# A fused attention, expert and gated-FFN kernel: operand sets of six up blocks made during the expert steps and kept in DRAM, a new order of units, and out weights split piece by piece

## The chip, the cores and the metric

The kernel runs on one core of a Trainium2 chip. A core has a matmul engine (TensorE, PE in the profile), VectorE (DVE), ScalarE (ACT), GpSimd (POOL) and SyncE (SP), which here only issues DMAs. The time is that of one launch in device microseconds; the runs shown give 937.08 us as the median of three (935.49 to 937.7).

## The reference

```
attn: phi(x) = [exp(p), exp(-p)], p = x @ w_phi - max|x @ w_phi|;  out = phi(q) (phi(k)^T v) / (phi(q) sum phi(k))
x     = attention's rows, 2304 x 512
moe:  e = argmax(x @ w_gate);  x = gate_w * sigmoid(x @ w_output_gate)[e] * (relu(x @ w1[e]) @ w2[e])
ffn:  xn = x / rms(x) * rms_g;  out = (silu(xn @ w_gate) * (xn @ w_val)) @ w_out       (512 -> 1536 -> 512)
```

Everything is float32. TensorE takes an operand as a rounded high part and a low part (`fp32r`), and each product of matrices is three matmuls: high by high, high by low and low by high.

## The kernel before, in words

Attention is first, the experts second. With these inputs the expert phase has eight steps of 288 rows on three experts. A step has eight chunks m of hidden rows: `hidden(m)` on TensorE, `relu` on ScalarE (the high part), `relu_low` on VectorE, and `outputs(m - 2)`. At the chunk m = 7 the rows of the next step are turned (`next_transpose`, four pieces) and split (`take_rows` on ScalarE and VectorE). `copy_out`, `add_squares`, `mean`, `root`, `inverse` and `normal` normalise a step's rows during the next step, and SP stores them into `xn_dram`. The first steps of an expert also split the next expert's weights.

The FFN's up part makes 12 blocks of 128 hidden columns for three groups of 768 rows, in 36 units (one block, one group). A unit is one two-by-two product made with seven products instead of eight; each product has six matmuls of 384 columns, so a unit has 42. For this the block's weights need four given parts and three sums, and a group's rows too. GpSimd makes the sums (`up_sums`, `up_last_sum`, `row_sums`), ScalarE rounds the high parts (`up_high`, `row_high`), VectorE subtracts for the low parts (`up_low`, `row_low`). TensorE does `product(u, 0)`, `(u, 1)`, `(u, 2)`, then the last product of unit u - 1, then `(u, 3)` to `(u, 5)`. ScalarE copies three sums per unit from PSUM (`first_copy`, L1418, before product 3 may start; `second_copy`, L1424, before product 5; `third_copy`, L1430, when product 5 is done) and computes two sigmoids (`first_sigmoid`, L1408; `second_sigmoid`, L1412). VectorE adds the gates and values and multiplies; SP stores the result (`hidden_out`, 384 KB).

A block's weights are loaded raw (512 KB, `up_in`, L568) into one of three staging buffers and split again each time the block comes up: 14 loads, in two operand buffers (`tH_up`, `tL_up`). Units go: blocks 0 and 1 with group 0, 0 and 1 with group 1, blocks 2 to 9 with all three groups each, blocks 10 and 11 by group, and blocks 0 and 1 again with group 2. Each engine's queue is an order written out by hand; an engine runs its queue in order, so whoever waits holds up all that stands behind it. SP's queue is one queue for loads and stores.

At the end the FFN's out weights (`out_high`, L1436; `out_low`, L1960) are split in two lumps of six, and 18 tiles of 128 rows are loaded, split and multiplied (L1188 to L1190).

Of the kernel before, what the change touches and what calls it, by code (L numbers as in the profile page):

```python
# [51 lines left out]
NQ = NF + 2  # L52
NT = NTOK // P
UNITS = ([(q, sg) for sg in range(2) for q in range(2)] + [(q, sg) for q in range(2, NF - 2) for sg in range(NSG)]
         + [(q, sg) for sg in range(NSG) for q in (NF - 2, NF - 1)] + [(NF, NSG - 1), (NF + 1, NSG - 1)])
NU = len(UNITS)


def unit_block(u):
    return UNITS[u][0] % NF  # L60


def first_of_pair(q):
    return min(u for u in range(NU) if UNITS[u][0] == q)


def last_of_pair(q):
    return max(u for u in range(NU) if UNITS[u][0] == q)
# [6 lines left out]
def last_of_group(sg):  # L75
    return max(u for u in range(NU) if UNITS[u][1] == sg)

# [5 lines left out]
def build_program(nc, q, k, v, w_phi, wg, wog, w1, w2, ffn_up, ffn_out, rms_g, out):  # L83
# [4 lines left out]
    xn_dram = nc.dram_tensor("xn_dram", [P, KC, NTOK + G], F32).ap()  # L88
    h_dram = nc.dram_tensor("h_dram", [P, NT, NF, P], F32).ap()
    ids_dram = nc.dram_tensor("ids_dram", [NTOK + G, 1], F32).ap()  # L90
    ctx = ExitStack()
    with ctx:
# [68 lines left out]
        put = placer(at_raw, RAW)  # L161
        tH_up, tL_up = [None, None], [None, None]
        tH_up[1] = put("upH1", [P, 7, 2, P], F32R)
        tL_up[1] = put("upL1", [P, 7, 2, P], F32R)
        xst = [put("xst0", [P, KC, 2 * GN]), None, None]
        xst[2] = xst[0]
        w_st = [put("w_st0", [P, 6, 2, P]), None, None]
        put = placer(at_work + 30368, WORK - 30368)
        tH_up[0] = put("upH0", [P, 7, 2, P], F32R)
        tL_up[0] = put("upL0", [P, 7, 2, P], F32R)  # L170
# [5 lines left out]
        w_st[1] = placer(at_work + 20032, 6144)("w_st1", [P, 6, 2, P])  # L176
        ysb = placer(at_work + 20032, 6144)("ysb", [P, 3, DM])

        PIECE = 2 * GN * 4

        def piece(n, count=1):
            return placer(at_set0 + n * PIECE, count * PIECE)

        own = ([*range(0, 10), *range(22, 26)], [*range(10, 22), 26, 27], [*range(28, 42)])
        sH = [[piece(own[sg][2 * o])(f"sH{sg}_{o}", [P, 2, GN], F32R) for o in range(7)] for sg in range(NSG)]
# [246 lines left out]
        def staging_of(q):  # L432
            return (0, 2)[q] if q < 2 else 1 - q % 2

        def loads_of(q):

            return 16 * len([n for n in range(q + 1) if staging_of(n) == staging_of(q)])
# [1642 lines left out]
```

## Time and profile before

| | us |
|---|---|
| median of 3 runs | 937.08 |
| the profiled execution, its own time | 927.2 |
| its span, first to last instruction | 925.6 |
| PE busy | 851.8 (92%) |
| DVE / ACT / POOL busy | 530.2 / 359.0 / 197.6 |
| DMA moved | 95.41 MB, mean 103 GB/s |

"Busy" is an average over stages. The digits of the page's second part show where TensorE isn't busy: slices of 23 us each, digits in tenths.

### The profile page before, as it was taken

The page shows a single profiled execution, that of the slowest core. Times are in us where ns is not written, and L with a number is a line of the kernel's source. Part 1 is how long each engine was busy: PE and PEld are TensorE (multiplying, and loading weights), DVE is VectorE, ACT ScalarE, POOL GpSimd, SP SyncE. Part 2 cuts the span into 40 slices and gives each one's busy share as a digit, 9 for nine tenths or more (in the row PEclk, how much of TensorE's full clock was granted, in tenths as well). Part 3 has the DMA queues.
Part 4 walks back from the last instruction along what each step waited for, and adds up shares of the span by engine and source line. Part 5 has one row for each costly group of instructions (what it writes and reads, how often), then busy time and mean ns, then how long its engine had stood idle before and what let it go on. Part 6 is the DMA issues. An engine that isn't in the chain of part 4 may idle for free.

```text
span 925.6 us, 16649 instructions
## 1 busy us (share of the span) xinstructions
PE 851.8 (92%) x6216; PEld 769.6 (83%) x6217; DVE 530.2 (57%) x931; ACT 359.0 (39%) x607; POOL 197.6 (21%) x211
## 2 busy tenths in 40 slices
PE   8999999999999999998672899999999678999997
PEld 6776868589999999998562799999999677888886
DVE  5688888998576333226664766666675484221220
ACT  4545555651454222224521543443443343222221
POOL 1011202034432122234604211111120120111011
PEclk9999999999999999999885999999999879999999
DMA  8615523023573212253007122222231623433430
GB/s 282 185 53 209 180 95 109 1 79 91 196 231 56 34 43 30 47 142 112 21 8 158 43 74 75 75 84 81 75 97 52 248 70 115 136 132 130 137 103 34
DMA packets 59755, 95.41 MB, mean 103 GB/s; under 512 B 8848, under 2 KB 42768, under 8 KB 57648
## 3 DMA queue, kind: packets, MB, share of 16 engines
q1 hardware_dynamic: 55392, 75.99, 28.5%
q0 software_dynamic: 3488, 17.85, 5.2%
q8 instruction: 37, 0.61, 0.3%
q10 hardware_dynamic: 816, 0.79, 0.3%
q14 instruction: 22, 0.18, 0.1%
HBM read 61.55 MB, written 33.08 MB: 102 GB/s over the span
## 4 chain that ended last, share of the span: by engine, by line
PE 76%; DVE 11%; issue 5%; DMA 3%; ACT 3%; POOL 1%; SPq 0%; POOLq 0%; ACTq 0%; DVEq 0%
PE ps L1138 8%; PE ps L1140 7%; PE ps L1139 7%; PE ps L1188 5%; PE ps L1190 5%; PE ps L1189 5%; PE ps L1049 4%; PE ps L1050 4%; PE ps L1051 4%; PE ps L1062 4%; PE ps L1064 4%; PE ps L1063 4%; PE ps L890 3%; PE ps L945 2%; PE ps L850 2%
## 5 line engine op out<-in xcount | busy, mean ns | idle before, releaser
L1138 PE MATMUL ps<-sH,upH 128*128 128x384 f32 x504 | 178.5, 354 | 53.9 <-ACT part L1424 28.7
L1139 PE MATMUL ps<-sL,upH 128*128 128x384 f32 x504 | 175.7, 349 | 0.0
L1140 PE MATMUL ps<-sH,upL 128*128 128x384 f32 x504 | 175.5, 348 | 0.0
L1138 PEld LDWEIGHTS ps<-sH,upH 128*128 128x128 f32 x504 | 99.7, 198 | 59.6 <-ACT part L1424 30.8
L1139 PEld LDWEIGHTS ps<-sL,upH 128*128 128x128 f32 x504 | 99.7, 198 | 0.1
L1140 PEld LDWEIGHTS ps<-sH,upL 128*128 128x128 f32 x504 | 99.4, 197 | 0.0
L1966 DVE TENSOR_TENSOR hTL<-h_st,hTH 128x768 fp32r<-128x768 f32 x36 | 32.9, 954 | 97.7 <-ACT hTH L1446 97.7
L1188 PE MATMUL ps<-woH,hTH 128*128 128x512 f32 x216 | 84.1, 389 | 2.4 <-DVE hTL L1966 2.4
L1742 DVE SCALAR_TENSOR_TENSOR hmL<-ps,hmH 128x288 fp32r<-128x288 f32 x64 | 29.2, 456 | 96.4 <-ACT hmH L1293 91.7
L1189 PE MATMUL ps<-woL,hTH 128*128 128x512 f32 x216 | 84.0, 389 | 0.0
L1190 PE MATMUL ps<-woH,hTL 128*128 128x512 f32 x216 | 84.0, 389 | 0.0
L1049 PE MATMUL ps<-xmH,w1H 128*128 128x288 f32 x256 | 76.0, 297 | 3.9 <-issue 2.0
L1062 PE MATMUL ps<-hmH,w2H 128*128 128x288 f32 x256 | 78.6, 307 | 0.0
L1050 PE MATMUL ps<-xmL,w1H 128*128 128x288 f32 x256 | 76.1, 297 | 0.0
L1051 PE MATMUL ps<-xmH,w1L 128*128 128x288 f32 x256 | 76.0, 297 | 0.0
L1064 PE MATMUL ps<-hmH,w2L 128*128 128x288 f32 x256 | 75.7, 296 | 0.0
L1063 PE MATMUL ps<-hmL,w2H 128*128 128x288 f32 x256 | 75.6, 296 | 0.0
L1293 ACT ACTIVATE hmH<-ps 128x288 fp32r<-128x288 f32 x64 | 26.3, 411 | 114.6 <-PE ps L1064 93.9
L1540 DVE TENSOR_REDUCE mx<-ps 128x4 f32<-128x512 f32 x72 | 49.2, 684 | 17.9 <-PE ps L852 17.7
L1547 DVE TENSOR_TENSOR pm<-ps,mx 128x512 f32<-128x512 f32 x72 | 49.8, 691 | 5.4
L1049 PEld LDWEIGHTS ps<-xmH,w1H 128*128 128x128 f32 x256 | 48.2, 188 | 4.7 <-issue 4.7
L1452 ACT ACTIVATE ysb<-ps 128x512 f32<-128x512 f32 x18 | 10.8, 598 | 105.8 <-PE ps L1190 105.8
(238 smaller groups left out, 1782.5 us busy)
## 6 DMA issues: line engine op xcount, KB each, us to landing
h_dram<-hid SPq DMA_DIRECT2D x36, 384.0 KB, 2.7
h_st<-h_dram SPq DMA_DIRECT2D x18, 768.0 KB, 4.2
w_st<-in_ffn_up SPq DMA_DIRECT2D x14, 512.0 KB, 4.5
xin<-xs_dram SPq DMA_DIRECT2D x9, 578.2 KB, 8.2
xs_dram<-zrow SPq DMA_DIRECT2D x8, 578.2 KB, 7.6
qT<-in_q SPq DMA_DIRECT2D x4, 1152.0 KB, 6.1
xn_dram<-x2g SPq DMA_DIRECT2D x8, 576.0 KB, 5.5
xst<-xn_dram SPq DMA_DIRECT2D x3, 1536.0 KB, 8.6
```

What stands on the lines that cost most here:

```text
L1049: e.matmul(o, w1H[par][:, c, cols], xmH[:, c, :], start=(c == 0), stop=False)
L1050: e.matmul(o, w1H[par][:, c, cols], xmL[:, c, :], start=False, stop=False)
L1051: last = e.matmul(o, w1L[par][:, c, cols], xmH[:, c, :], start=False, stop=(c == KC - 1))
L1062: e.matmul(o, w2H[par][:, m, cols], hmH[:, m % 2, :], start=(m == 0), stop=False)
L1063: e.matmul(o, w2H[par][:, m, cols], hmL[:, m % 2, :], start=False, stop=False)
L1064: last = e.matmul(o, w2L[par][:, m, cols], hmH[:, m % 2, :], start=False, stop=(m == FC - 1))
L1138: e.matmul(to, wh, xh, start=(fresh and c == 0), stop=False, skip_group_check=True)
L1139: e.matmul(to, wh, xl, start=False, stop=False, skip_group_check=True)
L1140: done = e.matmul(to, wl, xh, start=False, stop=(c == 1), skip_group_check=True)
L1188: e.matmul(to, hi, woH[:, i, :], start=(i == 0), stop=False, skip_group_check=True)
L1189: e.matmul(to, hi, woL[:, i, :], start=False, stop=False, skip_group_check=True)
L1190: done = e.matmul(to, lo, woH[:, i, :], start=False, stop=(i == NF - 1), skip_group_check=True)
```

## The change

An up block's operands, 1.75 MB with high and low parts, become a "set" in one of three buffers `tb[v % 3]`. A list `VISITS` names the block of each of 16 visits.

- Expert steps: each step after the first loads a block's raw weights (512 KB), makes three sums on GpSimd, one high part of 1792 elements on ScalarE (behind relu 5) and one low part on VectorE (behind relu_low 6), and SP stores the set (1.75 MB) to `t_dram`. With eight steps, steps 1 to 6 are stored: blocks 0 to 5. The last step makes a set that isn't stored.
- Up part: visits of blocks 0 to 5 load their set in two DMAs (1 MB, 0.75 MB). Six visits (6, 7, 8, 10, 11, 12) still load raw weights, into one staging buffer `w_st`, and make the set at units 11, 14, 17, 19, 22, 25 (`MADE_AT`).
- Order: units 0 to 3 are blocks 0 to 3 with group 0, units 4 to 6 blocks 1 to 3 with group 1, then blocks 4 to 8 with all groups, block 0 with groups 1 and 2, blocks 9 to 11 by group, and blocks 1 to 3 with group 2. Row operands are placed between copies by a table (`ROWS_AT`).
- Out weights are split one piece at a time from unit 30 on, and tile 0's rows in unit 34; their loads are issued at units 26 and 29.
- After the experts the sum of squares stands before product 2 of unit 1, and the root's function table is loaded once before all sigmoids.

```diff
+VISITS = (0, 1, 2, 3, 4, 5, 6, 7, 8, 0, 9, 10, 11, 1, 2, 3)
+MADE = (6, 7, 8, 10, 11, 12)
+MADE_AT = {6: 11, 7: 14, 8: 17, 10: 19, 11: 22, 12: 25}
+OUT_AT = {(30 + (n + 1) // 3, "ABC"[(n + 1) % 3]): n for n in range(NF)}
...
 (SP, in the loop over expert steps)
+                step_weights_in(n + 1)
                 rows_out(n)
+                weights_out(n + 1)
...
+            def step_weights_in(n):
+                e.wait_ge(s["e_st"], n * 16 + 16)
+                e.dma_start(t_raw[:, 0:4, :, :].rearrange("p o c n -> p (o c n)"), ffn_up[nth]...).then_inc(s["e_in"], 16)
+            def weights_out(n):
+                e.wait_ge(s["e_lo"], n + 1)
+                e.dma_start(t_dram[nth]..., tb[1][:, :, :, :, :]...).then_inc(s["e_st"], 16)
+            def weights_in(v):
+                if nth_made(v) > 0:
+                    e.wait_ge(s["t_lo"], 2 * nth_made(v))
+                else:
+                    e.wait_ge(s["s_lo"], 7 * NSG)
+                e.dma_start(w_st[:, 0:4, :, :]..., ffn_up[VISITS[v] + 1]).then_inc(s["w_in"], 16)
...
             for u in range(2, NU):
                 hidden_out(u)
+                for vis in range(4, len(VISITS)):
+                    if vis not in MADE and last_of_visit(vis - 3) == u + 1:
+                        operands_in(vis)
+                    if vis == MADE[0] and u == 8 or vis in MADE[1:] and u == MADE_AT[MADE[nth_made(vis) - 1]]:
+                        weights_in(vis)
...
 (ScalarE)
+            def weights_high(g):
+                e.wait_ge(s["e_add"], g * 3 + 3)
+                e.activation(tb[1][:, 0, :, :, :], t_raw[:, :, :, :], ACT.Copy).then_inc(s["e_hi"], 1)
+            def made_high(v, half):
+                slots, free = (slice(0, 4), slice(4, 7))[half], ("pe_U", "pe_D")[half]
+                e.wait_ge(s["t_add"], 3 * nth_made(v) + 3)
+                e.wait_ge(s[free], last_of_visit(v - 3) + 1)
+                e.activation(tb[v % 3][:, 0, slots, :, :], w_st[:, slots, :, :], ACT.Copy).then_inc(s["t_hi"], 1)
+            for u in range(2, NU):
                 first_copy(u)
                 first_sigmoid(u)
+                beside(u, "A")
                 second_sigmoid(u - 1)
                 second_copy(u)
+                beside(u, "B")
                 third_copy(u)
+                beside(u, "C")
```

Three places of ScalarE's queue follow. First, the second half of an expert step, before; `hmH` is a relu, `xmH` the next step's rows:

```order
L1293 ACTIVATE hmH<-ps 128x288
L1291 REGISTER_ALU
L1293 ACTIVATE hmH<-ps 128x288
L1286 ISA
L1287 ACTIVATE xmH<-ps 128x288
```

and in the changed kernel:

```order
L1380 ACTIVATE hmH<-ps 128x288
L1401 ISA
L1403 ACTIVATE tb_94<-t_raw 128x1792
L1378 REGISTER_ALU
L1380 ACTIVATE hmH<-ps 128x288
L1373 ISA
L1374 ACTIVATE xmH<-ps 128x288
```

The set's high part stands between relu 5 and relu 6, behind a wait for GpSimd. Second, the start of the up part, before (`upH` are weights, `sH` rows, `part` the copies, `hid` the sigmoids):

```order
L1310 ACTIVATE mx<-ones 128x1
L1384 ACTIVATE upH_97<-w_st_96 128x768
L1456 REGISTER_ALU
L1402 ACTIVATE sH_0_109<-xst_95 128x768
L1402 ACTIVATE sH_1_110<-xst_95 128x768
L1402 ACTIVATE sH_2_111<-s_sum_2_151 128x768
L1384 ACTIVATE upH_97<-w_st_96 128x768
L1418 ACTIVATE part_104<-ps 128x384
```

and in the changed kernel:

```order
L1486 ACT_TABLE_LOAD
L1486 ACTIVATE sH_0_109<-xst_97 128x768
L1486 ACTIVATE sH_1_110<-xst_97 128x768
L1486 ACTIVATE sH_2_111<-s_sum_2_151 128x768
L1486 ACTIVATE sH_3_112<-s_sum_3_152 128x768
L1384 ISA
L1386 ISA
L1388 ACTIVATE x2g<-ps 128x1152
L1502 ACTIVATE part_106<-ps 128x384
```

The weight operands are gone from the front; a table load is still there. Third, units 17 to 19 of the changed kernel, with the made sets of visit 8 (`tb_95`) and visit 10 (`tb_94`):

```order
L1473 ACTIVATE tb_95<-w_st 128x768
L1514 ACTIVATE part_108<-ps 128x384
L1502 ACTIVATE part_106<-ps 128x384
L1492 ACTIVATE hid_103<-gate_0_101 128x384
L1496 ACTIVATE hid_104<-gate_1_102 128x384
L1508 ACTIVATE part_107<-ps 128x384
L1514 ACTIVATE part_108<-ps 128x384
L1502 ACTIVATE part_106<-ps 128x384
L1492 ACTIVATE hid_104<-gate_1_102 128x384
L1473 ACTIVATE tb_94<-w_st 128x1024
L1496 ACTIVATE hid_103<-gate_0_101 128x384
L1508 ACTIVATE part_107<-ps 128x384
```

Only one unit, 18, lies between the two made sets; between the others lie two.

## Rows read from the trace of the kernel before

**Rows 1.** The page's slices of the span, TensorE's busy tenths.
```profile
PE   8999999999999999998672899999999678999997
```
**Rows 2.** Timeline of PE: start, us, line, what, idle time before it and its releaser.
```profile
435.03 0.44 PE L1138 MATMUL ps<-sH,upH 128*128 128x384 f32 x1 [3.51 <-DVE sL L1928]
...
448.25 0.69 PE L1138 MATMUL ps<-sH,upH 128*128 128x384 f32 x1 [2.58 <-DVE upL L1916]
...
453.60 0.34 PE L1140 MATMUL ps<-sH,upL 128*128 128x384 f32 x1
...
771.71 0.50 PE L1188 MATMUL ps<-woH,hTH 128*128 128x512 f32 x1 [2.44 <-DVE hTL L1966]
```
**Rows 3.** Timeline of ACT: third copies of units 6, 7, 31 and 35.
```profile
534.68 0.49 ACT L1430 ACTIVATE part<-ps 128x384 f32<-128x384 f32 x1 [1.32 <-PE ps L1140]
...
541.99 0.49 ACT L1430 ACTIVATE part<-ps 128x384 f32<-128x384 f32 x1 [1.59 <-PE ps L1140]
...
719.32 0.49 ACT L1430 ACTIVATE part<-ps 128x384 f32<-128x384 f32 x1 [1.59 <-PE ps L1140]
...
769.31 0.49 ACT L1430 ACTIVATE part<-ps 128x384 f32<-128x384 f32 x1
```
**Rows 4.** Timeline of SP's queue: stores of two steps' rows, a raw block's load.
```profile
396.56 0.62 SPq L547 DMA_DIRECT2D xn_dram<-x2g  x1
...
423.80 0.62 SPq L547 DMA_DIRECT2D xn_dram<-x2g  x1
...
487.86 0.35 SPq L568 DMA_DIRECT2D w_st<-in_ffn_up  x1
```
**Rows 5.** Timeline of ACT: the two waits for a load.
```profile
497.70 0.84 ACT L1384 ACTIVATE upH<-w_st 128x768 fp32r<-128x768 f32 x1 [18.43 <-DMA w_st<-in_ffn_up]
...
733.48 2.19 ACT L1436 ACTIVATE woH<-wo_st 128x512 fp32r<-128x512 f32 x4 [8.38 <-DMA wo_st<-in_ffn_out]
```
**Rows 6.** Timeline of SP's queue: a raw block is asked for after unit 31.
```profile
719.73 0.54 SPq L568 DMA_DIRECT2D w_st<-in_ffn_up  x1
```
**Rows 7.** Timeline of POOL: sums of 256 and 768 elements.
```profile
414.26 0.73 POOL L777 TENSOR_TENSOR w_st<-w_st 128x256 f32<-128x256 f32 x1
...
425.85 1.84 POOL L793 TENSOR_TENSOR s_sum<-xst 128x768 f32<-128x768 f32 x1 [9.36 <-PE ps L1051]
...
724.05 0.74 POOL L777 TENSOR_TENSOR w_st<-w_st 128x256 f32<-128x256 f32 x1 [28.96 <-DMA w_st<-in_ffn_up]
...
726.33 1.33 POOL L780 TENSOR_TENSOR w_st<-w_st 128x256 f32<-128x256 f32 x1
```
**Rows 8.** Timeline of ACT: the last expert step, the junction, unit 32's first sigmoid.
```profile
424.16 0.41 ACT L1293 ACTIVATE hmH<-ps 128x288 fp32r<-128x288 f32 x1 [2.81 <-PE ps L1064]
...
430.05 1.28 ACT L1310 ACT_TABLE_LOAD   x1 [1.15 <-issue]
...
431.46 0.83 ACT L1384 ACTIVATE upH<-w_st 128x768 fp32r<-128x768 f32 x1
...
442.11 0.41 ACT L1384 ACTIVATE upH<-w_st 128x256 fp32r<-128x256 f32 x1
...
722.38 0.52 ACT L1408 ACTIVATE hid<-gate 128x384 f32<-128x384 f32 x1 [1.51 <-DMA h_dram<-hid]
```
**Rows 9.** Timeline of DVE: the last expert step, and row operands beside GpSimd and alone.
```profile
426.40 0.82 DVE L1736 TENSOR_TENSOR xmL<-ps,xmH 128x288 fp32r<-128x288 f32 x2 [1.34 <-ACT xmH L1287]
...
441.87 2.40 DVE L1928 TENSOR_TENSOR sL<-s_sum,sH 128x768 fp32r<-128x768 f32 x1 [0.38 <-ACT sH L1402]
...
479.13 0.95 DVE L1928 TENSOR_TENSOR sL<-xst,sH 128x768 fp32r<-128x768 f32 x1
```
**Rows 10.** DMA issues of the window 395 to 545 us: count, size each, median us to landing.
```profile
xst<-xn_dram SPq DMA_DIRECT2D x3, 1536.0 KB, 8.6
...
xin<-xs_dram SPq DMA_DIRECT2D x1, 578.2 KB, 8.3
```
**Rows 11.** The stores into `xn_dram` (576 KB each), by that name: all eight.
```profile
DMA to landing us min/median/max: 3.4/5.6/13.6
```

More of the change, by code:

```diff
@@ L284, in build_program @@
             "normalised, stored; token numbers stored, read": "dve_xn xst idst id_in id_c",
+            "FFN up weights of a step: loaded, sums, operands split, stored": "e_in e_add e_hi e_lo e_st",
             "FFN rows loaded (one per group), their sums, operands split": "x_in0 x_in1 x_in2 s_add s_hi s_lo",
-            "FFN up weights loaded (one per staging buffer), their sums, operands split":
-                "w_in0 w_in1 w_in2 t_add t_hi t_lo",
+            "FFN up operands loaded (two parts per buffer)": "t_a0 t_a1 t_a2 t_b0 t_b1 t_b2",
+            "FFN up weights loaded, their sums, operands split (two parts each)": "w_in t_add t_hi t_lo",
             "a unit's products: the first, the second, sixth added, fifth added, fourth added": "pe_F pe_A pe_U pe_V pe_D",
@@ L431, in build_program, with step_number, nth_load, nth_made @@
         BANKS = ((2, 7, 0, 1), (3, 4, 5, 6))
[L432 to L437, printed above, removed]
-        def before_in_staging(q):
-            return max([n for n in range(q) if staging_of(n) == staging_of(q)], default=None)
+        SLOT = (0, 3, 2, 1, 5, 4, 6)
+        def step_number(g):
+            return nc.s_assert_within(g, 0, NSTEP - 1, skip_runtime_bounds_check_because="there are at most NSTEP steps")
+        def nth_load(v):
+            return len([n for n in range(v + 1) if n % 3 == v % 3 and n not in MADE])
+        def nth_made(v):
+            return MADE.index(v)
         def stores_of(u):
@@ L1777, in _ @@
                 take_rows(0, XT_FIRST)
-                for name in ("dve_ms", "dve_R", "dve_xn"):
+                for name in ("dve_ms", "dve_R", "dve_xn", "e_lo"):
                     e.sem_inc(s[name], 1)
@@ new lines, in beside @@
+            def beside(u, pos):
+                before = slot_before(u, pos)
+                if before in ROWS_AT:
+                    row_low(*ROWS_AT[before])
+                for vis in MADE:
+                    if before[0] == MADE_AT[vis] and before[1] != "C":
+                        made_low(vis, "AB".index(before[1]))
+                if before in OUT_AT:
+                    out_low(OUT_AT[before])
+                if before in TILE0_AT:
+                    tile_rows_low(0, TILE0_AT[before])
@@ new lines, in _ @@
+            for o in range(4):
+                row_low(0, o)
+            first_gate(0)
+            for o in range(4, 7):
+                row_low(0, o)
+            values(0)
+            first_gate(1)
+            mean(total - 1, BANKS[1][3])
+            second_gate(0)
+            inverse(total - 1)
+            hidden_rows(0)
+            values(1)
+            normal(total - 1)
+            for u in range(2, NU):
+                first_gate(u)
+                beside(u, "A")
+                second_gate(u - 1)
+                beside(u, "B")
@@ L2008, in _ @@
                 hidden_rows(u - 1)
                 values(u)
[L2010 to L2022 removed]
+                beside(u, "C")
@@ L2034, in _ @@
-                if u == NU - 1:
-                    for half in range(2):
-                        tile_rows_low(0, half)
             second_gate(NU - 1)
```

430 lines of the change are left out of this document (193 added, 237 removed).

## Prediction

> **What bounds the kernel now.** I read the slices first [rows 1]: TensorE is at 8 or 9 tenths everywhere but in two dents, slices 19 to 23 (the junction from the experts to the up part) and 32 to 34 (where the out weights come in). So the end is set by TensorE's work plus what it loses in the two dents, and what a change is worth there is read from the waits there.
>
> How much is lost: the third copies, one per unit right behind the unit's last sum, are a ruler [rows 3]. Units 6 and 7 lie 541.99 - 534.68 = 7.31 us apart, the length of an undisturbed unit (42 matmuls of 0.174). The experts' matmuls end at 435.03 - 3.51 = 431.5 [rows 2]. Unit 7's third copy could come eight units later, less the one product that is made in the next unit (1.04) and plus 0.1: 489.1. It comes at 541.99: 52.9 us are lost at the junction. From unit 7 to 31 it takes 177.3 for 24 x 7.31 = 175.4: 1.9 lost. From 31 to 35, 50.0 for 29.2: 20.8 lost. The first tile then waits 2.4 [rows 2]. In all 78.0 us.
>
> What the waits are: at the front TensorE waits 3.5 for VectorE's first low parts of rows. Its restart at 448.25 after 2.58 idle runs on the low level of the clock, 1.2 GHz: the 16 matmuls from there to 453.60 take 5.35 us, where 0.174 each and 0.25 for a restart make 3.0: 2.3 us lost [rows 2]. I use 2.3 for each wait of over 2.5 us. The largest is 18.4 us of ScalarE for block 2's raw weights [rows 5]: their load is issued only at 487.86 [rows 4], since in SP's queue it stands behind the store of the last normalised rows, with nothing for TensorE to do. In the second dent ScalarE waits 8.4 us for the out weights [rows 5] with copies queued behind it.
>
> **The change, part by part.**
>
> *Junction.* Four units on group 0 (29 us of work) now stand before group 1, and nine units (66 us) before group 2; blocks 0 to 3 come ready from DRAM. The 18.4 us wait and those for later groups have no cause left, if the loads come. Chain at the front: the table load at 430.05 stays, so the first high part of rows starts where `upH` starts now, 431.46, takes 0.83, and VectorE's low part 0.95 alone [rows 8, 9]: TensorE starts at about 433.35, 1.85 late instead of 3.5. Product 4 of unit 0 waits for its low part beside `add_squares` on GpSimd, where such a subtraction takes up to 2.40 instead of 0.95 [rows 9]: 0.7, and product 5 again 0.6. In unit 1 the matmuls of the squares take 0.3, and ScalarE has a root with its table, another table (1.28 each [rows 8]) and two sigmoids before the second copy: 1.0. In unit 2 VectorE is behind by `inverse` and `normal`: 0.6. One more for units 3 to 8, where row operands are slotted in. Sum 6.05, all short waits, so I put no clock on them: 6.0 instead of 52.9.
>
> The loads behind this: a set of 1.75 MB is 1.17 times a group of rows, 1536 KB in 8.6 us [rows 10], so about 10 us alone. Sets 1 and 2 are asked for at about 427.5 and 428.5, group 1 at 431.5, set 3 at 436 and 442. Even one after the other at 8 to 10 us each they are there at 437, 446, 455 and 463, where unit 1 starts at 441, unit 2 at 449, unit 3 at 457 and group 1 (unit 4) at 464. Set 3 is behind group 1 and would be late by up to 6 us on this count; but landing times include a fixed part that overlapped DMAs don't pay again, so I take 0 and keep 6 + 2.3 for a rival.
>
> *Expert steps.* Per step GpSimd gets sums of 512, 256 and 256 elements: 1.28 (between 0.73 for 256 and 1.84 for 768 [rows 7]) + 0.73 + 0.73 = 2.8. ScalarE gets 1792 elements: 0.41 for 256 and 0.83 for 768 [rows 8] give 1.67, in the 2.8 us that it waits between two relus [rows 8]: covered. VectorE gets 1792 x 0.95 / 768 = 2.2 at most, from 425.1 on, half a us behind ScalarE's relu 6 [rows 8]: it runs to 427.2, over the place of the next rows' low parts at 426.40 [rows 9], which then end 0.7 later, and TensorE's third and fourth transposes need those. I find 0.2 of stall per step, seven steps, 1.4; in the two steps that also split the next expert's weights there is less room, 0.8 each: 3.0. Bounds: 0 (the relus have several us of slack), and 2.2 x 7 = 15.4 if each subtraction passes whole.
>
> The ring `t_raw`, sums, high, low, store, next load must fit a step of 27.2 (the stores of two steps' rows, 396.56 and 423.80 [rows 4]). Store 1.75 MB: from 9 us (group load, scaled) to 17 (the 576 KB store of 5.6 [rows 11] times 3.1); load 4.3 [rows 6, 7]; 2.8; 1.7; 2.2: 20 to 28. I take 20, since the stored rows are long pieces as in the group's load, and the 576 KB store has short ones. The rows' load of 8.3 us [rows 10] stands behind the store, and is still there before GpSimd gates it.
>
> By the Trainium skill (DMA: Bandwidth & Descriptors, Anatomy of one DMA) a DMA's semaphore waits for the receipt of the last byte from the target memory, which takes longest for HBM; this speaks for the long end of the ring. The store of 576 KB at 5.6 us [rows 11] agrees with a slow store; by that rule alone the expert term would be larger by the rival B below.
>
> *Middle.* A set made in the up part needs: load issued at the end of unit E, sums, then the high part in slot A of a later unit. Now: issue 719.73, about 0.5 behind unit 31's end (719.2); sums from 724.05 to 727.66 [rows 6, 7]. So 8.5 behind the end; with 512 elements in the first sum 9.0. Slot A of the next unit is right behind the first sigmoid, 722.90 [rows 8], 3.7 behind the end; of the one after, 11.0. All sets but one are asked for two units ahead: 2.0 to spare. Visit 10 is asked for behind unit 18 and made in unit 19, with slot A at 3.7: ScalarE waits 5.3, then the high part of 1024 elements (1.0), the second sigmoid and the second copy (0.45 each): the copy is ready 11.0 behind the end of unit 18, where product 5 of unit 19 wants it at 6.3 (six products of 1.05). TensorE loses 4.7 and 2.3 for the clock, 7.0. Bounds 0 and 9.3. The 1.9 of small things stays.
>
> On the clock the Trainium skill (TensorE: Matmul & The Clock Gate, Part 1) says that the number of cold matmuls varies between runs of one kernel. The rows above show 16; by the rule the 7.0 would be anything from 4.7 up to 7.0.
>
> *Second dent.* Out weights are asked for at unit 26 (3 MB) and split one by one from unit 30, 0.55 and 0.62 us each, in gaps: ScalarE's and VectorE's work per unit grows to 4.2 and 5.9 of 7.31. Tile 0 is split in unit 34. What is left: the stores of hidden rows queue behind the 3 MB, and a first sigmoid waits for such a store already (1.51 [rows 8]): 1.5. Instead of 20.8 + 2.4. Bounds 0 and 8.
>
> *Sum.* Lost after: 6.0 + 1.9 + 7.0 + 1.5 + 3.0 = 19.4; before 78.0. Gain 58.6. The profiled execution 927.2 - 58.6 = 868.6. The median shown is 9.9 us or 1.07% above that execution; in proportion this gives 878.
>
> **The rivals.**
>
> A. As summed: 878 us.
>
> B. The ring or VectorE's subtraction reaches into each step. For it: VectorE is at the transposes' limit; for seven steps nothing catches up. Against: the slack of the relus. 2 to 3 us more per step, or a set that is late at the junction (8.3): 878 + 17 = 895.
>
> C. Visit 10 is in time, or the wait is swallowed: for it, sums alone take 2.8 instead of 3.6. Against: even that gives the copy at 0.5 + 4.3 + 2.8 + 1.0 + 0.9 = 9.5, where 6.3 is due; it needs more. 878 - 7 = 871, with no cost in the steps 868.
>
> D. Slower: the ring decides the step. From 27.2 us on each us goes into six steps; the gain is eaten when the ring takes 37 us, that is when store and load together land 30 us after issue. If the store scales like the slowest of its kind (13.6 us for 576 KB [rows 11] would be 42), the ring is 53 and the time 878 + 6 x 26 = 1034. Against: the store's long rows.
>
> E. It doesn't do what it says: the waits only move from the weights to the rows, since sums, splits and stores of the last step stay as they are. If half of what I take off the junction stays (23.5), 902; if all stays, no change, 937.
>
> **How the numbers follow.** A 0.52, B 0.22, C 0.15, D 0.03, E 0.08 (of which 0.01 no change). The time is A's, 878. The range takes B and C in and stops before E: 863 to 898. A measurement of this kernel can tell about 0.2% from no change. Faster 0.95, same 0.01, slower 0.04.
>
> **What would show it.** In the changed profile: a slice row without the first dent; the third copies 7.3 apart from unit 2 on but for one gap of 14 at unit 19, with ScalarE's longest wait "DMA w_st" or "POOL w_st" there; relus in the expert steps still 3.2 apart and steps of 27.2; the first matmul of the up part 1.9 behind the last of the experts; the first tile's matmul right behind unit 35. Steps of over 28 us would show B; matmuls waiting for `tb` loads, a late queue; a junction with waits for `sL`, E.

## The result, and the profile after

The changed kernel takes 901.87 us (median of 4 runs, 901.04 to 903.25) where the kernel before takes 936.29 (932.16 to 937.7): ratio 0.9641, 95% interval 0.9607 to 0.9674. It is faster, by 34.4 us and not by the 59 forecast, and 901.9 lies outside the range of 863 to 898. Its profiled execution took 903.25 us, with a span of 901.5.

The page's slices of the changed kernel (TensorE, then its granted clock) answer to [rows 1]:

```profile
PE   8999999999998899999898899998999999999997
PEclk9999999999999999999989999998999999999999
```

The two dents are gone as deep ones; what is left are single tenths at many places: slices 13, 14 and 17 in the expert steps, 20, 22 and 23 around the junction, 28 at units 19 and 20. Who is waited for, in PE's waits (us in all, times, longest):

```profile
PE ps L1225 <- ACT part L1508: 14.5, 8, 3.8
PE ps L1225 <- DVE sL L1991: 7.0, 4, 3.4
PE ps L1098 <- DVE xmL L1792: 3.7, 2, 2.4
```

The largest is the second copy of a unit, eight times, none longer than 3.8. Such a list names only the last link, so I go by the ruler of [rows 3] again. ScalarE's timeline has the first table load, with which the expert steps begin, and the third copies of units 7, 31 and 35; PE's has the first matmul of the up part:

```profile
245.64 1.28 ACT L1397 ACT_TABLE_LOAD   x1 [2.77 <-issue]
526.35 0.49 ACT L1514 ACTIVATE part<-ps 128x384 f32<-128x384 f32 x1 [0.68 <-PE ps L1227]
712.96 0.49 ACT L1514 ACTIVATE part<-ps 128x384 f32<-128x384 f32 x1 [1.06 <-PE ps L1227]
747.84 0.49 ACT L1514 ACTIVATE part<-ps 128x384 f32<-128x384 f32 x1 [1.59 <-PE ps L1227]
```

```profile
448.98 0.45 PE L1225 MATMUL ps<-sH,tb 128*128 128x384 f32 x1 [1.88 <-DVE sL L1991]
```

The experts end at 448.98 - 1.88 = 447.10. Unit 7 could come 57.5 us later (the count of the prediction), at 504.6, and comes at 526.35: 21.7 lost. From 7 to 31 it takes 186.6 for 175.4, from 31 to 35 34.9 for 29.2. From the table load to the experts' end it takes 201.5 us; before it was 431.5 - 238.4 = 193.1. Term by term:

| us lost | predicted | profile after |
|---|---|---|
| junction, to unit 7 | 6.0 | 21.7 |
| small things, units 8 to 31 | 1.9 | 2.8 |
| visit 10 at units 19 and 20 | 7.0 | 6.5 |
| second dent (unit 29: 1.9, units 32 and 33: 5.7) | 1.5 | 7.6 |
| expert steps | 3.0 | 8.4 |
| sum | 19.4 | 47.0 |

Before's second profile (b0_again below) has 194.5 us of expert steps instead of 193.1, and five profiles of after have 199.4 to 202.5, so the 8.4 is 5 to 9.

What each of them is, in the timelines. The rows of the expert steps come first: VectorE's low part of the six blocks, then its low part of the next step's rows, for which TensorE's last transposes wait.

```profile
301.01 2.01 DVE L1931 TENSOR_TENSOR tb<-t_raw,tb 128x1792 fp32r<-128x1792 f32 x1
302.94 0.81 DVE L1792 TENSOR_TENSOR xmL<-ps,xmH 128x288 fp32r<-128x288 f32 x2
303.53 0.96 PE L1098 MATMUL ps<-ident,xin 96*128 96x96 f32 x6 [2.37 <-DVE xmL L1792]
```

Unit 0, at the junction, loses 7.0 us: its third copy comes 13.3 us behind the experts' end instead of 6.4. TensorE waits 1.88, 1.17 and 0.52 us for low parts of rows, while VectorE works beside GpSimd's last sum of group 0 (1.82 us alone, 2.59 here). And it runs on the low level of its clock: 18 matmuls start 0.32 us apart, where 0.174 is usual. The last line is the stretch of 447 to 461 us (busy times, then granted clock 0.76, DMA share, GB/s):

```profile
448.04 2.59 POOL L886 TENSOR_TENSOR s_sum<-xst 128x768 f32<-128x768 f32 x1
447.97 3.47 DVE L1991 TENSOR_TENSOR sL<-xst,sH 128x768 fp32r<-128x768 f32 x2 [2.88 <-issue]
451.50 0.69 PE L1225 MATMUL ps<-sH,tb 128*128 128x384 f32 x1 [1.17 <-DVE sL L1991]
447.00:461.00 14.00, 10.43 (x42) 9.13 (x42) 11.71 (x9) 7.70 (x12) 8.93 (x5) 0.76 0.85 295
```

Over the whole junction (447.10 to 526.35) TensorE stands idle for 13.0 us, and 49 matmuls are 0.32 us apart instead of 0.174. That is about 7 us (estimate: 49 x 0.146), so a third of the 21.7 is the clock.

Unit 2 loses 5.1: GpSimd's sums of group 1 stand beside VectorE's hidden rows and normalisation, and ScalarE waits for a gate behind them. VectorE's multiplication of hidden rows, 0.96 us alone, takes 2.48, and the normalisation's four instructions take 3.90.

```profile
467.40 2.67 POOL L882 TENSOR_TENSOR s_sum<-s_sum,xst 128x768 f32<-128x768 f32 x1
468.40 2.48 DVE L2019 TENSOR_TENSOR hid<-hid,val 128x768 f32<-128x768 f32 x1
471.86 3.90 DVE L1819 SCALAR_TENSOR_TENSOR x2g<-x2g,gcol,rinv 128x288 f32<-128x288 f32 x4
476.26 0.52 ACT L1492 ACTIVATE hid<-gate 128x384 f32<-128x384 f32 x1 [6.41 <-DVE gate L1997]
478.36 0.69 PE L1225 MATMUL ps<-sH,tb 128*128 128x384 f32 x1 [2.96 <-ACT part L1508]
```

Unit 4: SyncE asks for row group 2 (1536 KB) at 481.00, and the 384 KB store of unit 2's hidden rows follows at 488.62. ScalarE's first sigmoid of unit 4 may only overwrite that buffer once the store has landed, 7.1 us later; such a store takes 2.9 us in the median. The last line is the busy share, in tenths, of the DMA engines from 486 to 497 us, in slices of 0.275:

```profile
481.00 0.58 SPq L628 DMA_DIRECT2D xst<-xn_dram  x1
488.62 11.64 SPq L633 DMA_DIRECT2D h_dram<-hid  x2
495.76 0.52 ACT L1492 ACTIVATE hid<-gate 128x384 f32<-128x384 f32 x1 [5.72 <-DMA h_dram<-hid]
498.15 0.41 PE L1225 MATMUL ps<-sH,tb 128*128 128x384 f32 x1 [3.41 <-DVE sL L1991]
DMA  9999996310000999990000000000000000000000
```

The load isn't what the store waits for: the load lands 7.7 us after its issue, at 488.7, as the store is issued. The store's packets move from 489.6 to 491.2, then the engines are all but idle until it counts as landed at 495.76. Between load and store stands one more DMA, in every kernel here: the store of the last step's token numbers (`ids_dram`, 1.1 KB in pieces of 4 B, issued at 481.93), which itself lands late (10.7 us in a0_again). In before the hidden store issued right behind it (485.22 and 485.88) took 11.0 us, the longest of all there. Whether it delays the hidden stores was not tested.

Unit 6 isn't such a case either. ScalarE waits 4.83 us there, but the store is issued only at 511.53, 3.2 us behind unit 5's third copy (508.36), since VectorE is late beside GpSimd's sums of group 2, and it lands in 3.1 us like any other.

```profile
511.53 0.37 SPq L633 DMA_DIRECT2D h_dram<-hid  x1
514.72 0.52 ACT L1492 ACTIVATE hid<-gate 128x384 f32<-128x384 f32 x1 [4.83 <-DMA h_dram<-hid]
```

Unit 32 is a store behind loads: a set (`tb`) and two tiles' hidden rows (`h_st`) stand before it, the DMA engines are busy all the time, and it lands after 8.0 us. Unit 29, behind the 3 MB of out weights, is the smaller case (6.5 us).

```profile
705.99 4.39 SPq L614 DMA_DIRECT2D tb<-t_dram  x2
710.51 0.99 SPq L643 DMA_DIRECT2D h_st<-h_dram  x2
712.97 0.37 SPq L633 DMA_DIRECT2D h_dram<-hid  x1
721.07 0.52 ACT L1492 ACTIVATE hid<-gate 128x384 f32<-128x384 f32 x1 [6.58 <-DMA h_dram<-hid]
722.95 0.44 PE L1225 MATMUL ps<-sH,tb 128*128 128x384 f32 x1 [3.78 <-ACT part L1508]
```

Unit 19 is the wait that was predicted: the raw weights of visit 10 are asked for at the end of unit 18, and ScalarE waits 4.38 for their sums.

```profile
609.57 0.54 SPq L624 DMA_DIRECT2D w_st<-in_ffn_up  x1
617.12 1.06 ACT L1473 ACTIVATE tb<-w_st 128x1024 fp32r<-128x1024 f32 x1 [4.38 <-POOL w_st L873]
619.02 0.69 PE L1225 MATMUL ps<-sH,tb 128*128 128x384 f32 x1 [3.56 <-ACT part L1508]
```

### The profile page after: what moved, and what is told of

Same layout as the page of the kernel before. It is cut to its first block, busy times and chain, and to the rows that moved or that the text cites. A ratio compares the mean times of both kernels' runs of the same rounds, so it can differ in the third digit from the quotient of the medians.

```text
span 901.5 us, 16661 instructions
## 1 busy us (share of the span) xinstructions
PE 851.4 (94%) x6216; PEld 767.9 (85%) x6217; DVE 527.1 (58%) x908; ACT 354.3 (39%) x583; POOL 186.0 (21%) x194
## 4 chain that ended last, share of the span: by engine, by line
PE 76%; DVE 10%; issue 6%; DMA 4%; ACT 2%; POOL 0%; DVEq 0%; POOLq 0%; SPq 0%; ACTq 0%
PE ps L1225 8%; PE ps L1227 7%; PE ps L1226 7%; PE ps L1277 5%; PE ps L1276 5%; PE ps L1275 5%; PE ps L1133 4%; DMA h_dram<-hid 4%; PE ps L1134 3%; PE ps L1135 3%; PE ps L1146 3%; PE ps L1148 3%; PE ps L1147 3%; PE ps L974 3%; PE ps L1029 3%
## 5 line engine op out<-in xcount | busy, mean ns | idle before, releaser
L1225 PE MATMUL ps<-sH,tb 128*128 128x384 f32 x504 | 175.6, 348 | 23.2 <-ACT part L1508 14.5
L1227 PE MATMUL ps<-sH,tb 128*128 128x384 f32 x504 | 173.4, 344 | 0.0
L1226 PE MATMUL ps<-sL,tb 128*128 128x384 f32 x504 | 173.2, 344 | 0.0
L1225 PEld LDWEIGHTS ps<-sH,tb 128*128 128x128 f32 x504 | 97.9, 194 | 28.8 <-ACT part L1508 21.1
L1226 PEld LDWEIGHTS ps<-sL,tb 128*128 128x128 f32 x504 | 97.8, 194 | 0.1
L1227 PEld LDWEIGHTS ps<-sH,tb 128*128 128x128 f32 x504 | 97.5, 193 | 0.0
L1380 ACT ACTIVATE hmH<-ps 128x288 fp32r<-128x288 f32 x64 | 26.3, 411 | 105.0 <-PE ps L1148 84.2
L904 POOL DMA_INDIRECT out_dram<-ysb,idI x18 | 17.4, 967 | 219.1 <-ACT ysb L1536 219.1
## 6 DMA issues: line engine op xcount, KB each, us to landing
t_dram<-tb SPq DMA_DIRECT2D x6, 1792.0 KB, 11.1
xin<-xs_dram SPq DMA_DIRECT2D x9, 578.2 KB, 11.4
```

The source lines that it names most:

```text
L1225: e.matmul(to, wh, xh, start=(fresh and c == 0), stop=False, skip_group_check=True)
L1226: e.matmul(to, wh, xl, start=False, stop=False, skip_group_check=True)
L1227: done = e.matmul(to, wl, xh, start=False, stop=(c == 1), skip_group_check=True)
```

## The experiments

All times are in this table: medians with the lowest and highest run, the ratio to the kernel before with its 95% interval, and from each profile the ruler's losses (junction, units 8 to 31, second dent from unit 31 on) and the length of the expert steps. Kernels of one set ran on one chip; the difference to "after" counts within a set.

| set, kernel | us | ratio to before | steps | junction | 8 to 31 | from 31 |
|---|---|---|---|---|---|---|
| 0 after | 901.9 (901.0 to 903.3) | 0.964 (.961 to .967) | 201.5 | 21.7 | 11.2 | 5.6 |
| 1 after (a0) | 892.5 (890.9 to 893.2) | 0.956 (.953 to .959) | 200.0 | 15.8 | 9.0 | 5.7 |
| 1 stores on ScalarE's queue (e1) | 916.2 (913.5 to 920.6) | 0.983 (.979 to .987) | 199.3 | 26.3 | 14.0 | 12.7 |
| 1 visits 6, 7, 8 sooner (e4) | 896.8 (894.5 to 897.7) | 0.961 (.958 to .964) | 200.7 | 18.2 | 8.1 | 6.4 |
| 2 after (a1) | 899.1 (896.2 to 903.0) | 0.964 (.959 to .968) | 199.4 | 20.8 | 12.0 | 6.1 |
| 2 visit 8 sooner (e4b) | 898.9 (896.3 to 902.8) | 0.962 (.959 to .965) | 202.2 | 21.0 | 12.8 | 5.7 |
| 2 no row sums (e5) | 895.1 (892.9 to 896.3) | 0.958 (.955 to .961) | 201.0 | 14.9 | 10.7 | 6.7 |
| 2 loads in pieces (e6) | 890.8 (887.7 to 891.4) | 0.953 (.950 to .957) | 201.6 | 17.8 | 8.8 | 0.9 |
| 3 after (a2) | 898.5 (893.6 to 900.3) | 0.961 (.958 to .964) | 202.5 | 16.6 | 11.9 | 6.0 |
| 3 low parts behind rows (e2) | 893.4 (888.3 to 895.0) | 0.956 (.952 to .959) | 195.6 | 18.3 | 9.3 | 5.5 |
| 3 raw loads one unit sooner (e9) | 889.5 (887.6 to 890.6) | 0.952 (.950 to .955) | 200.4 | 16.8 | 3.2 | 5.4 |
| 3 four edits (e12) | 875.0 (874.5 to 879.8) | 0.939 (.937 to .942) | 195.6 | 16.0 | 1.4 | 0.2 |
| 4 after (a3) | 894.4 (893.9 to 897.7) | 0.956 (.954 to .959) | 199.8 | 17.4 | 9.3 | 7.6 |
| 4 3 KB stores (e13) | 895.7 (891.8 to 896.6) | 0.957 (.953 to .961) | 200.4 | 15.9 | 6.4 | 6.6 |
| 4 four edits (e12b) | 878.9 (875.5 to 881.4) | 0.941 (.937 to .944) | 195.6 | 16.3 | 1.3 | 0.3 |
| 4 four edits, 3 KB stores (e14) | 876.2 (872.4 to 878.2) | 0.936 (.932 to .939) | 195.7 | 14.8 | 0.9 | 0.7 |
| 5 e1 with 3 KB stores (e15) | 892.5 (889.9 to 896.2) | 0.957 (.954 to .960) | 199.9 | 21.8 | 7.0 | 4.8 |
| 5 e12 with these (e17) | 883.7 (881.5 to 887.1) | 0.948 (.944 to .952) | 195.7 | 18.7 | 6.0 | 2.8 |

**The same kernels again.** The attention stage, whose code is unchanged, was 7.3 us longer in the profile after.

> The kernel before, unchanged, profiled a second time. In the two profiles the expert steps begin at 238.4 us (before) and 245.6 us (after), though the attention stage is the same code. Theory 'chance': the attention stage differs from one execution to the next, so the expert steps begin here anywhere from 238 to 246 us, and the profiled execution takes 927 to 937 us. Rival 'the change costs 7 us in the attention stage' (another layout of the program): they begin at 238 to 239 us again and the profiled execution takes about 927 us.

> The kernel after, unchanged, profiled and timed a second time. Theory 'chance': the expert steps begin somewhere from 238 to 246 us, the rest of the profile (expert steps 200 us, junction 21.5 us lost, second dent 7.5 us lost) repeats within 1 us each; time 902. Rival 'the change costs 7 us in the attention stage': they begin at 245 to 246 us again.

The kernel before, profiled again, took 934.87 us, and its expert steps begin at 244.66:

```profile
244.66 1.28 ACT L1310 ACT_TABLE_LOAD   x1 [2.76 <-issue]
```

In the profiles of the kernel after they begin at 245.6, 243.4, 243.4, 245.5 and 245.9, in all other kernels below between 243.3 and 248.4. So the 7 us aren't the change, and the profile of before that the prediction rests on was a short one. The kernel after itself is less steady than I expected: medians of 892.5 to 901.9 us in five sets of runs, each spread over 2 to 7 us, where before has medians of 932.4 to 936.3 in six.

> The kernel after once more, on the same chip as the three kernels sent with it. It took 901.9 us in one set of runs and 892.5 us in another. Theory 'sets of runs differ': anywhere from 890 to 903 us, and the gaps between third copies at units 4, 6, 19, 29 and 32 repeat within 2 us each. Rival 'one of the two sets was an exception': 892 us again.

> The kernel after once more, for the comparison with the three kernels sent with it. It has taken 892.5, 899.1 and 901.9 us in three sets of runs, while the kernel before took 933.6, 934.0 and 936.3. All theories: 890 to 903 us.

> The kernel after, for the comparison with the three kernels sent with it: 890 to 903 us by all theories.

The part that differs most is the junction (15.8 to 21.7), and next the second expert step (28.5 to 31.4 us; before has 27.2 and 28.6). In the junction 2.5 us are unit 0: its third copy comes 13.3 us behind the experts' end in after and a1_again, and 10.8 in the other three. There GpSimd's last sum of group 0 is over as VectorE begins, TensorE's two further waits of 1.17 and 0.52 are one of 0.51 to 0.55, and 14 to 16 matmuls run on the low level of the clock instead of 18. So one profile of each kernel can't tell a difference of 2 or 3 us at the junction.

**Hidden stores on another queue (e1).** The store and its wait move from SyncE's queue to ScalarE's:

```
 second_sigmoid(u - 1) ... third_copy(u); beside(u, "C")
+hidden_out(u - 1)          # was SyncE's
```

> After, with the stores of the hidden rows issued on ScalarE's queue, behind the third copy, instead of on SyncE's, where they stand behind loads of 0.8 to 1.8 MB. Theory 'one queue': ScalarE's waits for a hidden store at units 4, 6, 29 and 32 (5.7, 4.8, 5.0, 6.6 us) shrink to the 3 us that a store takes alone, and with them PE's losses there (4.3, 2.5, 1.9 and 5.7 us): 888 to 892 us. Rival 'the DMA engines themselves are full': the stores land as late from another queue, since the same 16 engines carry the loads: 899 to 903 us. Second rival 'the loads are only the last of several lateness': the store lands early, but VectorE is late there (it runs beside GpSimd), and PE waits as long for another engine: 895 to 902 us.

All three accounts missed: 916.2 us, 23.7 slower than after in its set. The load of group 2 in SyncE's queue, the store, and what waits for it:

```profile
473.36 0.57 SPq L628 DMA_DIRECT2D xst<-xn_dram  x1
474.23 0.38 ACTq L1489 DMA_DIRECT2D h_dram<-hid  x1
486.79 0.52 ACT L1484 ACTIVATE hid<-gate 128x384 f32<-128x384 f32 x1 [10.26 <-DMA h_dram<-hid]
488.89 0.69 PE L1217 MATMUL ps<-sH,tb 128*128 128x384 f32 x1 [7.59 <-ACT part L1506]
```

Issued 0.9 us behind one load, the store lands 12.5 us later, worse than any in SyncE's queue (at most 8.8 in five profiles of after). "One queue" falls: another queue is no way past a load. The Trainium skill says as much (DMA: Bandwidth & Descriptors, Issuing engines are not separate DMA queues): DMAs run on the same 16 DMA engines and interleave, whoever starts them. The trace agrees. But e1 changes an order too. This is unit 1's store, which SyncE's queue issues 0.6 us ahead of the load in after (480.40 and 481.00), where it lands in 3.3 us; with the store on ScalarE's queue nothing holds the load back for it. The 23.7 us are the price of the other queue and of the order that came with it, and no run separates the two.

**Loads in pieces (e6).** If the bytes under way count, fewer at a time help:

```
-group_in(2)
+group_in(2, rows 0:2) ... hidden_out(2); group_in(2, rows 2:4)
-unit 26: wo_st thirds 0, 1, 2      unit 29: hidden_in(0), hidden_in(1)
+units 26, 27, 28: one third each   units 32, 33: one tile each
```

> After, with SyncE's large loads spread among the hidden stores: row group 2 in two halves (before and behind the store of unit 2), the out weights in thirds at units 26, 27 and 28 instead of all at 26, the first two tiles' hidden rows at units 32 and 33 instead of both at 29. Theory (formed after the store from ScalarE's queue had landed 12.5 us late beside one load): a 0.4 MB store takes as long as the bytes that are under way with it, so only fewer bytes at a time help; losses at units 4, 29, 32 and 33 fall from about 10 us to 3 us: 6 to 7 us below the kernel after of this call. Rival 'the bytes are the same and the queue is full anyway': within 1.5 us of the kernel after.

890.8 us, 8.3 less than after in its set, and no run of the one overlaps one of the other. Unit 32's third copy follows 7.6 us after unit 31's instead of 12.6, unit 29's 7.3 instead of 9.3; unit 4 gains only 0.9 (12.2 to 11.3). The first sigmoid of unit 32:

```profile
710.24 0.53 ACT L1492 ACTIVATE hid<-gate 128x384 f32<-128x384 f32 x1 [2.85 <-DMA h_dram<-hid]
```

2.85 us instead of 6.58, which a unit hides. The ruler loses 0.9 from unit 31 on and nothing at unit 29, 7.2 less than after: that settles the second dent. At unit 4 it speaks against the bytes ahead of the store: only half of the group stands there, its transfer is over 1.5 us before the store is issued, and the store still takes 5.8 us.

**Small packets or bytes (e13, e14, e15, e17).** A hidden store writes six stretches of 512 B per partition; with the DRAM tensor laid out by block first, one of 3 KB:

```
-h_dram [P, NT, NF, P]
+h_dram [P, NF, NT, P]
```

> After, with the hidden rows' tensor in DRAM laid out by block and then tile (it was tile and then block), so that one hidden store writes one stretch of 3 KB per partition in place of six of 512 B; the loads of the out stage still read 512 B pieces. Theory 'small packets': the store alone lands in under 2.4 us instead of 2.9, and beside a load it no longer takes 7 to 12 us: units 4, 6, 29 and 32 lose 5 us less in all, 5 us below the kernel after of this call. Rival 'bytes under way': a store behind a load in the queue waits for the load's bytes whatever its own packets are: within 1.5 us of the kernel after.

> The kernel of four edits with the hidden stores in 3 KB stretches. Theory 'small packets': units 4 and 6, which still lose 2.6 and 1.6 us there, lose under 1 us each: 871 to 873 us. Rival 'bytes under way': within 1 us of the kernel of four edits of this call.

The store lands in 2.4 us instead of 3.0 in the median, but the longest takes 9.2, and the kernel is no faster (895.7 for 894.4). In SyncE's own queue the packets make no difference, as the rival said. e14 is 2.7 us below e12b with runs that overlap; I count it as no difference. On a queue of its own it is otherwise:

> As the kernel with hidden stores on ScalarE's queue (916 us, one store 12.5 us late beside the load of row group 2), and its stores in 3 KB stretches instead of 512 B ones. Theory 'small packets': two queues share each DMA engine packet by packet, so a store of 512 B packets gets a small share beside a load of 3 to 7 KB packets; with packets of 3 KB the store lands within 5 us beside a load, and the time falls from 916 to 890 to 897 us. Rival 'a load already under way keeps the engines': the longest wait of ScalarE for a store stays over 9 us and the time over 910 us.

> The kernel of four edits with its hidden stores on ScalarE's queue and in 3 KB stretches. Theory 'small packets': stores no longer stand behind any load, units 4 and 6 lose under 1 us each: 870 to 874 us. Rival 'a load already under way keeps the engines': 885 us or more.

e15 takes 892.5 us where e1 took 916.2 in another set, with the same order and bytes. ScalarE's waits for stores fall from 93.3 us to 49.4. These are the busy share of the DMA engines (slices of 0.55 us) and the DMA issues of e1 and then of e15 in the window 470 to 492 us (KB each, median us to landing):

```profile
DMA  0099910067699999999981220200000000000000
xst<-xn_dram SPq DMA_DIRECT2D x1, 1536.0 KB, 9.7
h_dram<-hid ACTq DMA_DIRECT2D x2, 384.0 KB, 7.6
```

```profile
DMA  0000008991006798999899981000000000000000
xst<-xn_dram SPq DMA_DIRECT2D x1, 1536.0 KB, 12.4
h_dram<-hid ACTq DMA_DIRECT2D x1, 384.0 KB, 11.1
ids_dram<-xs_dram SPq DMA_DIRECT2D x1, 1.1 KB, 11.7
```

So small packets explain most of e1's loss, as the time says, but not this one store beside group 2, which takes 11.1 us with 3 KB packets too. The same page of the Trainium skill has a rule that fits the first half (Queues, rings and completion order): each DMA engine goes round its queues a packet at a time. No run here shows the share that a queue gets. Why the store beside group 2 is as late is open. The DMA engines are all but idle from about 481.5 us in e1 and 483.5 in e15, yet the store lands at 486.7 and 487.9; in both the token numbers' store was issued beside it and, in e15, lands 0.3 us later. e17 is 7.5 us over e14 in another set: on the kernel of four edits ScalarE's queue is the worse place, and both accounts of its expectation missed (870 to 874, 885 or more).

**When the raw weights are asked for (e4, e4b, e9).**

```
e4:  -MADE_AT = {6: 11, 7: 14, 8: 17, ...}   +{6: 10, 7: 13, 8: 16, ...}
e4b: +{6: 11, 7: 14, 8: 16, ...}
e9:  -u == MADE_AT[visit made before]         +u == MADE_AT[visit made before] - 1
```

> After, with the three first visits whose sets are made on chip (6, 7, 8) made at units 10, 13 and 16 instead of 11, 14 and 17, so that the raw weights of visit 10 are asked for one unit sooner. Theory: ScalarE's wait of 4.4 us for GpSimd's sums at unit 19 goes, and units 19 and 20 lose nothing instead of 6.5 us: 895 to 896 us. Rival 'the load is late for another reason' (the sums themselves, or loads of sets in the same queue): the wait stays, 902 us. Second rival: the wait moves to unit 10, where the first raw weights now have 1.5 units from request to use: 898 to 902 us.

> After, with only visit 8's sets made sooner (unit 16 instead of 17); visits 6 and 7 stay at 11 and 14. Theory: the raw weights of visit 10 are asked for one unit sooner, the wait at unit 19 goes, and no wait comes at unit 10, where making visit 6 sooner had cost 5 us: 5 us less than the kernel after of this call. Rival 'the wait moves again', to unit 16, which has two units from the request of visit 8's raw weights to their use: within 1.5 us of the kernel after.

> After, with each raw load of a block made on chip asked for one unit sooner (behind the hidden store of the unit before), the units in which the sets are made unchanged. Theory: from request to use there are then three units everywhere and the wait at unit 19 goes without coming back at unit 16 or 10: 5 to 6 us less than the kernel after of this call. Rival 'the loads delay the hidden stores': units 14, 17, 22 and 25 lose 1 us or more each, and the gain is 2 us or less.

Times in brackets are from one third copy to the next, where 7.3 is an undisturbed unit. In e4 the wait at unit 19 goes (11.1 to 7.3) and comes back at units 10 and 11 (11.4 and 8.3); in e4b it comes back at units 16 and 17 (12.9 and 8.7). Both are the rival in which the wait moves, and neither kernel is faster; e4 is 4.3 us slower than after in its set. In e9, where only the request moves, it is gone and nothing takes its place: units 19 and 20 lose 0.0 instead of 5.1, 889.5 us, 9.0 below after in its set. SyncE's request and GpSimd's last sum for visit 10 in e9:

```profile
598.92 0.34 SPq L624 DMA_DIRECT2D w_st<-in_ffn_up  x1
605.00 0.73 POOL L873 TENSOR_TENSOR w_st<-w_st 128x256 f32<-128x256 f32 x1
```

The sums are ready at 605.7, unit 18's third copy comes at 603.4, and slot A of unit 19 about 4 us behind it. Two units from request to use are too few, three enough. Of the 9.0 us, 5.1 are units 19 and 20 and 1.5 smaller waits at units 14 and 17; units 29 and 30 (2.0) and the second expert step (1.8) differ as much between two sets of after.

**GpSimd beside VectorE (e5).** GpSimd's row sums write 8 columns instead of 384, and the parts made from them read the loaded rows instead, so this kernel leaves the sums' values out of the product:

```
-tensor_tensor(to[5][:, :, :], x[:, 0:2, GN:2 * GN], x[:, 2:4, GN:2 * GN], add)
+tensor_tensor(to[5][:, :, 0:8], x[:, 0:2, GN:GN + 8], x[:, 2:4, GN:GN + 8], add)   # and so the other three
-src = s_sum[sg][o]
+src = x[:, 2 * (o % 2):2 * (o % 2) + 2, 0:GN]
```

> After, with GpSimd's sums of the rows (12 of 128x768) cut to 8 of 384 columns each, and the parts that need the sums made from the loaded rows instead, so that their values are left out of the product. Theory 'shared port': VectorE's instructions at the junction that take 1.6 to 3.5 us beside GpSimd take 0.95 us, and units 0, 2 and 6 lose 8 us less in all: 8 us below the kernel after of this call. Rival 'the order is what costs': the hidden rows are still stored and loaded late, ScalarE still waits for a gate behind the normalisation: at most 3 us below.

895.1 us, 4.0 below after in its set, and the junction loses 14.9 instead of 20.8. That is between the two accounts. Of the 5.9, unit 0 gains 2.5, unit 2 2.1, units 5 and 6 2.1, and unit 4 loses 1.0 more, where the store waits as before. The 2.5 of unit 0 are also missing in three of the five profiles of after, whose sums are over in time, and against those e5 loses only 0.9 to 2.5 less. So GpSimd's sums are a part of the junction's loss, 4 us by the time, and not the most of it.

**VectorE's order in the expert steps (e2).**

```
-if m == 6: weights_low(g)
 take_rows(g + 1, XT_BANK, (2, 3))
+weights_low(g)
```

> After, with VectorE's low parts of the six blocks (2.0 us in each expert step) moved behind the step's last rows' low parts, for which PE waits to begin the next step. Theory 'order on VectorE': in the first two steps with six-block work PE's waits for VectorE's xmL at their end (1.3 and 1.9 us) go with the lower clock that follows them, and the first two steps take 28 us and less in place of 30.3 and 29.4: 4 us less than the kernel after of this call. Rival 'VectorE's whole load is too much beside the split of the next expert's weights': the wait goes to the pieces of that split or to the next step's first low parts, and the steps stay above 29 us: within 1.5 us.

893.4 us, 5.1 below after in its set. The three long steps take 29.0, 28.2 and 27.9 us instead of 30.3, 30.7 and 29.2, in the later sets too: 195.6 in all instead of 199 to 202. The wait for `xmL` is gone. A part of the rival holds in the first step, where TensorE now waits for the last piece of the next expert's weights:

```profile
274.08 2.02 DVE L1931 TENSOR_TENSOR tb<-t_raw,tb 128x1792 fp32r<-128x1792 f32 x1
276.02 1.22 DVE L1738 TENSOR_TENSOR w2L<-w2raw,w2H 128x1024 fp32r<-128x1024 f32 x1
277.72 0.39 PE L1133 MATMUL ps<-xmH,w1H 128*128 128x288 f32 x1 [1.55 <-DVE w2L L1738]
```

**The four edits together (e12, e12b)**: e2, e6, e9, and the normalisation of the last rows moved behind the gates of unit 1 and 2.

> After, with four edits together: VectorE's low parts of the six blocks behind the rows, the raw loads one unit sooner, SyncE's loads in pieces, and the normalisation of the last expert rows behind the gates of units 1 and 2 instead of ahead of them. Theory 'the terms add': 4 + 6 + 8 us, and 3 us at unit 2: 20 us less than the kernel after of this call, 874 to 881 us. Rival 'they share their cause': waits removed in one place come up in the next (the first units are late for several engines at once): 8 to 14 us less, 884 to 891 us.

> The kernel of four edits once more; it took 875.0 us when the kernel after took 898.5. All theories: 873 to 880 us.

875.0 us where after takes 898.5, and again 878.9 where it takes 894.4: 23.5 and 15.5 less, and 6.1% and 5.9% below the kernel before. In the first set the terms add: alone e2, e6 and e9 gave 5.1, 8.3 (in another set) and 9.0. The 15.5 of the second set lies between the two accounts. The slices of e12, and PE's longest waits in the up part:

```profile
PE   8999999998999999999988899999999999999997
```

```profile
PE ps L1225 <- DVE sL L1990: 6.2, 2, 3.9
PE ps L1225 <- ACT part L1508: 2.5, 5, 0.8
```

Only the junction is left in the up part, with 16.0 us, 7.2 of them at unit 0, 2.7 at unit 2 and 2.6 at unit 4. The 3.9 at its front is new: in the last step VectorE's low part of the six blocks now stands ahead of the first rows' low parts, and TensorE waits 3.9 where it waited 1.88. The moved normalisation shows no gain that can be told from chance: unit 2 takes 10.0 and 11.0 us, in e2 without it 10.2.

## Why the prediction was wrong

The forecast of a faster kernel by its mechanism was right: the waits for raw weights at the junction and for out weights are gone, the first matmul of the up part is 1.88 late (1.85 predicted), the first tile follows with no wait, and unit 19 lost 6.5 us for 7.0. Four things were wrong, and they close the sum. The profile after is 34.7 us over the forecast for it (903.25 for 868.6); the terms above make 27.6 of it and the attention stage 7.3.

- **Junction, 6.0 for 21.7 (15.8 to 21.7 over five profiles).** The sum of 6.05 had 3.15 for unit 0, 1.3 for unit 1, 0.6 for unit 2 and 1.0 for units 3 to 8. The profile after has 7.0, 0.6, 5.1 and 9.1 (units 3 to 7). Two steps failed. First, "all short waits, so I put no clock on them": unit 0 waits 3.6 us, nearly as forecast, but the clock falls at these short waits, and its low level makes about 7 of the 21.7. It falls there in all five profiles of after. Second, VectorE was taken to be 0.6 us behind at unit 2 and 1.0 in all of the units after it. It is far more behind: the gate of unit 2 stands behind the hidden rows and the normalisation, slowed beside GpSimd, and unit 6's store is issued 3.2 late. e5 puts 4 us on the sums. A third term had no place in the sum at all: unit 4 loses 4.3 to a hidden store that lands late, and the prediction never asked how late a store may land. Moving the normalisation (e12) and halving the load (e6) each gained too little to tell from chance. In the kernel of four edits 16.0 are still lost; how VectorE's order shares it with the late store stays open.
- **Second dent, 1.5 for 7.6.** The stores behind the 3 MB were named and sized by a wait of 1.51 that was seen under lighter traffic [rows 8]; before's longest hidden store took 11.0 us, which no row of the prediction shows. The bound of 8 held. The worst one is not behind the out weights but behind a set and two tiles' rows at unit 32; e6 takes 7.2 us off by spreading the loads.
- **Expert steps, 3.0 for 8.4.** The mechanism was right (VectorE's low part ahead of the next rows), the size was not. "0.8 each in the two steps that also split" came out as 2.8 and 4.2 in this profile (the second of them had 1.4 us more in before's second profile too), and the fifth step as 1.2; the others lost nothing, not 0.2. The error is that the slack of a plain step was used for a split one, of which the rows showed none. e2 gives back 5.1.
- **From the profile to the median.** 9.3 us were added in proportion, since before's profile was short. That was nearly right for a wrong reason: 7.3 of it lie ahead of the expert steps and do not scale. So the miss of 23.9 us is 27.6 for the terms and 7.3 for the attention stage, less the 9.3 that were added and 1.4 by which this profile lies over its median.

The rivals: B (the ring, or VectorE's subtraction, reaches into each step) had the right place for a part, steps over 28 us, and its second cause is the one that e2 shows, though in three steps of seven and at half of B's 17 us. No step waited for the ring's loads, since the store's 11.1 us leave room in 27. E named the junction's waits for rows and had 902, the time that came, at a chance of 0.08; but half of them being left was not worked out from anything in the queue, and the 902 was reached by four terms, only one of them at that place. C and D did not happen.

The range was too narrow because the bounds of the single terms were kept (8 for the second dent, 9.3 for unit 19, 15.4 for the steps) and the junction, the largest, had none above 8.3.

## What to carry to other kernels

When a change lets loads run ahead, list for each queue what is issued behind every large load and who may not overwrite its buffer until it lands: a 0.4 MB store took 3 us alone and 6.5 to 9 behind 1.8 to 3 MB, and the cure was to spread the loads, not another queue. Then look whether the DMA engines are busy while such a store is under way: at unit 4 they weren't, and spreading the load gained 0.9. And price the clock's low level on short waits too: at unit 0 waits of 1.88, 1.17 and 0.52 us went with 18 slow matmuls. When a deadline is missed by one unit, move the request and not the deadline; moving the use only moved the wait. And profile both kernels twice before terms of a few us are trusted: one stage of unchanged code differed by 7 us between executions.

## What was not expected of the hardware

- A store issued on a second queue 0.9 us behind a 1536 KB load took 12.5 us, the last 5 of them with all but idle DMA engines. Issued ahead of that load, on the first queue, the same store took 3.3. With 3 KB packets instead of 512 B ones that whole kernel went from 916.2 to 892.5 us.
- VectorE's instruction on two SBUF operands of 128x768 took 0.95 us alone and up to 2.89 beside GpSimd, and GpSimd's own sum went from 1.85 to 3.66 us.
- The kernel before takes 932 to 936 us in every set, the kernel after 892 to 902. Between its slowest and fastest profile lie 11.7 us: 2.3 in the attention stage, 1.5 in the expert steps, 5.9 at the junction and 2.2 in units 8 to 31. Of the 5.9, 3.1 are idle time and the rest is mostly the clock's low level (49 matmuls against 34).
